# The first expert of mixture 1 split into two parts around the other seven, and a due table for two experts

## The reference

```python
x = attn_ref(x, weight).reshape(14336, 192)
# mixture 1
logits = x @ w_gate;  expert_idx = argmax(logits, 1);  gate_w = softmax(logits)[expert_idx]
for e in range(8):
    mask = expert_idx == e
    out[mask] = gate_w[mask, None] * (maximum(x[mask] @ w1[e], 0) @ w2[e])
# mixture 2, on the out of mixture 1
noisy = logits + log1p(exp(x @ w_noise)) * noise;  top2 = two largest;  top2_w = softmax over the two
for e in range(8):
    for k in range(2):
        mask = top2[:, k] == e
        out[mask] += top2_w[mask, k, None] * (maximum(x[mask] @ w1[e], 0) @ w2[e])
```

## Time and profile before

| | |
|---|---|
| median of 3 runs | 1960.8 us (1959.62 to 1962.15) |
| the profiled execution's own time | 1964.21 us |
| its span, first to last instruction | 1962.2 us |
| mean granted TensorE clock | 0.982 of full speed |
| TensorE matmuls busy | 1876.2 us, 96% of the span |
| VectorE / ScalarE / GpSimd busy | 1269.1 / 914.0 / 967.7 us |

### The profile page before, as it was taken

The page is one execution under the profiler, slowest core; times in us unless marked ns, Lnnn a source line. Parts: engine busy times, 40 slices in busy tenths (PEclk is TensorE's granted clock), DMA queues, the critical chain, the costliest instruction groups (busy, mean ns, idle before and its releaser), DMA issues.

```text
span 1962.2 us, 51451 instructions
## 1 busy us (share of the span) xinstructions
PE 1876.2 (96%) x14089; PEld 1821.5 (93%) x14090; DVE 1269.1 (65%) x4251; ACT 914.0 (47%) x2420; POOL 967.7 (49%) x1471
## 2 busy tenths in 40 slices
PE   8977599999999999799999999999999999999998
PEld 6657599999999999799999999999999999999998
DVE  5775488788887887655655655655655655655555
ACT  5543345555555455434444444444444444444444
POOL 4888554444444444444444444444444444444444
PEclk9979799999999999899999999999999999999999
DMA  7634243232332332322222222322322322322221
GB/s 274 230 113 128 74 127 120 89 115 79 117 118 84 116 100 92 103 74 62 81 78 62 85 74 62 104 63 63 102 62 64 96 64 66 97 62 86 78 63 48
DMA packets 113487, 185.23 MB, mean 94 GB/s; under 512 B 21675, under 2 KB 87971, under 8 KB 111287
## 3 DMA queue, kind: packets, MB, share of 16 engines
q1 hardware_dynamic: 73383, 104.53, 17.9%
q0 software_dynamic: 39936, 79.95, 12.6%
q10 hardware_dynamic: 144, 0.49, 0.1%
HBM read 111.34 MB, written 77.66 MB: 96 GB/s over the span
## 4 chain that ended last, share of the span: by engine, by line
PE 81%; issue 5%; DVE 5%; POOL 5%; ACT 1%; DMA 1%; DVEq 1%; ACTq 0%; POOLq 0%; SPq 0%
PE bank L1168 26%; PE bank L1169 12%; PE bank L1151 7%; PE bank L1153 7%; PE bank L1149 7%; PE bank L1152 7%; PE bank L1150 7%; POOL rows_of_mixture L1253 4%; PE bank L1138 2%; PE bank L1012 1%; DVE h_l L857 1%; PE bank L1139 1%; PE bank L1088 1%; POOL pause L1255 1%; DVE w1ml L666 1%
## 5 line engine op out<-in xcount | busy, mean ns | idle before, releaser
L1168 PE MATMUL bank<-w2hl,h_h 128*128 128x384 f32 (+1 forms) x2832 | 863.5, 370 | 14.4 <-DVE w2hl L672 6.7
L1169 PE MATMUL bank<-w2hl,h_l 128*128 128x192 f32 (+1 forms) x2832 | 721.1, 255 | 0.0
L857 DVE SCALAR_TENSOR_TENSOR h_l<-bank,h_h 128x512 fp32r<-128x512 f32 x708 | 477.5, 689 | 140.5 <-ACT h_h L565 101.2
L565 ACT ACTIVATE h_h<-bank 128x512 fp32r<-128x512 f32 x708 | 422.9, 598 | 301.2 <-PE bank L1153 261.6
L1168 PEld LDWEIGHTS bank<-w2hl,h_h 128*128 128x128 f32 x2832 | 534.0, 189 | 20.1 <-issue 12.6
L1169 PEld LDWEIGHTS bank<-w2hl,h_l 128*128 128x128 f32 x2832 | 543.1, 192 | 0.0
L1149 PE MATMUL bank<-x_h,w1mh 128*128 128x256 f32 x1416 | 401.7, 284 | 12.2 <-issue 9.5
L1280 POOL DMA_INDIRECT rows_of_mixture<-x_in,pos x248 | 245.7, 991 | 322.6 <-DVE h_l L857 110.0
L1151 PE MATMUL bank<-x_h,w1ml 128*128 128x256 f32 x1416 | 402.3, 284 | 0.5 <-issue 0.4
L1152 PE MATMUL bank<-x_h,w1lh 128*128 128x256 f32 x1416 | 400.1, 283 | 0.5 <-issue 0.5
L1153 PE MATMUL bank<-x_h,w1ll 128*128 128x256 f32 x1416 | 399.4, 282 | 0.2 <-issue 0.2
(11 more groups left out here) (199 smaller groups left out, 2017.0 us busy)
## 6 DMA issues: line engine op xcount, KB each, us to landing
rows<-rows_of_mixture SPq DMA_DIRECT2D x179, 208.0 KB
raw<-in_w_of_both SPq DMA_DIRECT2D x17, 1024.0 KB
raw<-in_w_of_both SPq DMA_DIRECT2D x17, 768.0 KB
out<-zeros SPq DMA_DIRECT2D x61, 192.0 KB
x_in<-in_x SPq DMA_DIRECT2D x15, 768.0 KB
raw<-in_moe_w_turned SPq DMA_DIRECT2D x8, 768.0 KB
rows_of_mixture<-pad_rows SPq DMA_DIRECT2D x21, 208.0 KB, 9.2
rows_of_mixture<-x_in,pos POOLq DMA_INDIRECT x248
```

Source lines behind the costliest of these rows:

```text
L565: nc.scalar.activation(h_h[:, 2 * p:2 * p + 2, :].rearrange("p c t -> p (c t)"), bank[1 + p][:], ACT.Relu).then_inc(hh_ready[m], 1)
L857: V.scalar_tensor_tensor(h_l[:, 2 * p:2 * p + 2, :].rearrange("p c t -> p (c t)"), bank[1 + p][:], 0.0, h_h[:, 2 * p:2 * p + 2, :].rearran ...
L1168: T.matmul(dst, h_h[:, c, tok], both, start=(c == 0), stop=False)
L1169: last = T.matmul(bank[5 + a][:, 0:width], h_l[:, c, tok], w2hl[:, c, 0:width], start=False, stop=(c == F // P - 1))
```

## The change

Mixture 1 is run in 9 parts instead of 8 experts (`PARTS = [E + 1, E]`). Part 0 is expert 0's first slots, at most four (`FIRST_SLOTS`) and at most all but one; parts 1 to 7 are the experts 1 to 7; part 8 is the rest of expert 0. With the counts above part 0 has 4 slots and part 8 has 2, so the number of slots stays 61. All engines loop over parts, and the running number of a set of weights becomes `PART0[m] + e`; expert 0's `w1` and `w2` are loaded and split a second time, for part 8. SP finds a part's first row in a new table `part_row`. `tables(0)` writes 9 entries instead of 8 and needs a fourth step in its running sum. The due table has a row for expert 0 and one for expert 1, so that SP waits for `slot_scattered` for the slots of both; the slots of part 2 and later still wait for all chunks.

```diff
+EARLY_EXPERTS = 2
+FIRST_SLOTS = 4
+PARTS = [E + 1, E]
+PART0 = [0, E + 1]
...
-                with sp_.Fori(0, E) as e:
+                def row_of(part, highest):
+
+                    if m == 1:
+                        return part * CAP
+                    return sp_.value_load(part_row[0:1, bass.ds(part, 1)], min_val=0, max_val=highest)
+
+                with sp_.Fori(0, PARTS[m]) as e:
...
-                                with sp_.If(e * WORD + j < EARLY - 1):
-                                    slot_scattered((j + 1) % EARLY)
+                                with sp_.If(e // EARLY_EXPERTS * WORD + j < EARLY - 1):
+                                    slot_scattered((e * E + j + 1) % (EARLY_EXPERTS * E))
...
-                            load_rows(e * CAP + j * SLOT + SLOT)
+                            load_rows(row_of(e, (E - 1) * CAP) + j * SLOT + SLOT)
                         with sp_.Else():
                             if m == 0:
-                                all_scattered()
+                                with sp_.If(e < 1):
+                                    slot_scattered(E)
+                                with sp_.Else():
+                                    all_scattered()
...
-                            load_rows((e + 1) * CAP)
-                        g = E * m + e
+                            load_rows(row_of(e + 1, E * CAP))
+                        g = PART0[m] + e
+                        following = (e + 1) % E + e // E * (E - 1) if m == 0 else (E + e + 1) % (2 * E)
                         with sp_.If(j < 1):
                             until((w1_ready, PAIRS * g + PAIRS))
-                            load_w1((g + 1) % (2 * E))
+                            load_w1(following)
...
-                    V.tensor_copy(first_count[:, k:k + 1], bank[2][0:1, RANKS:RANKS + 1])
+                    V.tensor_copy(first_count[:, :, k], bank[2][0:1, RANKS:RANKS + EARLY_EXPERTS])
...
+                parts = PARTS[m]
                 V.tensor_tensor(pad_at[m][:, 0:E], t_cnt[:], ecap[0:1, :], ALU.add)
-                V.memset(pad_at[m][:, E:E + 1], E * CAP).then_inc(pads_known[m], 1)
+                if m == 0:
+                    V.tensor_scalar(pad_at[m][:, E:E + 1], t_cnt[:, 0:1], float(SLOT), None, ALU.add)
+                V.memset(pad_at[m][:, parts:parts + 1], E * CAP).then_inc(pads_known[m], 1)
...
+                if m == 0:
+                    V.tensor_copy(part_row[:, 0:E], ecap[0:1, :])
+                    V.memset(part_row[:, E + 1:E + 2], E * CAP)
+                    V.tensor_scalar(slots[:, 1:E], t_shift[:, 1:E], 1.0, None, ALU.max)
+                    V.tensor_scalar(slots[:, E:E + 1], t_shift[:, 0:1], -float(FIRST_SLOTS), 1.0, ALU.add, ALU.max)
+                    link(V.tensor_scalar(t_first[:], t_shift[:, 0:1], -1.0, 1.0, ALU.add, ALU.max))
+                    link(V.tensor_scalar(slots[:, 0:1], t_first[:], float(FIRST_SLOTS), None, ALU.min))
+                    V.tensor_scalar(part_row[:, E:E + 1], slots[:, 0:1], float(SLOT), None, ALU.mult)
```

More of the change, by code:

```diff
@@ L61 @@
 WORD = 64
-C_TOTAL = E
+C_TOTAL = E + 1
 def empty_tiles(c):
@@ L154, in attention_and_two_mixtures @@
         c_pos = sb("c_pos", [TILE, XROW, CHUNK], i32)
-        slots_in = sb("slots_in", [1, E])
-        first_count = sb("first_count", [1, DUE_COLUMNS])
+        slots_in = sb("slots_in", [1, EARLY_EXPERTS, E])
+        first_count = sb("first_count", [1, EARLY_EXPERTS, DUE_COLUMNS])
         slot_full = sb("slot_full", [1, E])
-        slot_in = sb("slot_in", [1, DUE_COLUMNS, E])
+        slot_in = sb("slot_in", [1, EARLY_EXPERTS, DUE_COLUMNS, E])
         late = sb("late", [1, 1], i32)
-        due = sb("due", [1, E], i32)
+        due = sb("due", [1, EARLY_EXPERTS * E], i32)
         count2 = sb("count2", [P, SUBS, E], bf16)
-        one = [sb(f"one_{m + 1}", [1, E + 2], i32) for m in range(2)]
+        one = [sb(f"one_{m + 1}", [1, E + 3], i32) for m in range(2)]
         t_cnt = sb("t_cnt", [1, E])
         t_int, t_shift = sb("t_int", [1, E], i32), sb("t_shift", [1, E], i32)
-        t_word = sb("t_word", [1, E])
-        t_cum = sb("t_cum", [1, 3, 2 * E + 1])
-        pad_at = [sb(f"pad_at_{m + 1}", [1, E + 1], i32) for m in range(2)]
+        t_word = sb("t_word", [1, E + 1])
+        t_cum = sb("t_cum", [1, 3, 2 * E + 3])
+        t_first = sb("t_first", [1, 1])
+        part_row = sb("part_row", [1, E + 2], i32)
+        pad_at = [sb(f"pad_at_{m + 1}", [1, E + 2], i32) for m in range(2)]
         raw1 = sb("raw1", [P, 2, F])
@@ L356, in _ @@
                 else:
-                    sp_.wait_ge(late_ready, E)
+                    sp_.wait_ge(late_ready, PARTS[0])
                     missing = sp_.value_load(late[0:1, 0:1], min_val=0, max_val=1)
@@ L590, in body @@
                         if last:
-                            split_w1_h(E * m + e + 1, p)
+                            split_w1_h(PART0[m] + e + 1, p)
                         if p == 0 and m == 0:
@@ L618, in _ @@
                 total = total_of(act, m)
-                with act.Fori(0, E) as e:
+                with act.Fori(0, PARTS[m]) as e:
                     start, more = slots_of(act, m, e)
@@ L752, in early_slots @@
                 link = Steps(dve, dve_due)
-                shape = [1, DUE_COLUMNS, E]
+                shape = [1, EARLY_EXPERTS, DUE_COLUMNS, E]
                 link(V.tensor_scalar(slot_full[:], expert[0:1, :], float(SLOT), float(SLOT), ALU.mult, ALU.add))
-                link(V.tensor_tensor(slot_in[:], bc(first_count[:].unsqueeze(2), shape), bc(slot_full[:].unsqueeze(1), shape), ALU.is_ge))
-                link(V.reduce_sum(slots_in[:], slot_in[:].rearrange("p k j -> p j k"), AX.X))
-                V.tensor_scalar(due[:], slots_in[:], -1.0, float(CHUNKS), ALU.mult, ALU.add).then_inc(due_ready, 1)
+                link(V.tensor_tensor(slot_in[:], bc(first_count[:].unsqueeze(3), shape), bc(slot_full[:].unsqueeze(1).unsqueeze(1), shape), ALU.is_ge))
+                link(V.reduce_sum(slots_in[:], slot_in[:].rearrange("p s k j -> p s j k"), AX.X))
+                V.tensor_scalar(due[:], slots_in[:].rearrange("p s j -> p (s j)"), -1.0, float(CHUNKS), ALU.mult, ALU.add).then_inc(due_ready, 1)
             gate_to_low()
@@ L793, in tables @@
                 link(V.tensor_scalar(t_shift[:], t_int[:], SLOT.bit_length() - 1, None, ALU.arith_shift_right))
-                slots = t_cum[:, 0, E + 1:]
-                link(V.tensor_scalar(slots, t_shift[:], 1.0, None, ALU.max))
-                for i, step in enumerate((1, 2, 4)):
-                    a, b = t_cum[:, (0, 1, 2)[i], :], t_cum[:, (1, 2, 1)[i], :]
-                    link(V.tensor_tensor(b[:, E:], a[:, E:], a[:, E - step:2 * E + 1 - step], ALU.add))
-                before_e = t_cum[:, 1, E:]
@@ L800, in tables @@
-                link(V.scalar_tensor_tensor(t_word[:], before_e[:, 0:E], float(WORD), slots, ALU.mult, ALU.add))
-                V.tensor_scalar(one[m][:, 0:E], t_word[:], -1.0, None, ALU.add)
-                V.tensor_scalar(one[m][:, C_TOTAL + 1:C_TOTAL + 2], before_e[:, E:E + 1], -1.0, None, ALU.add)
-                V.tensor_copy(one[m][:, C_TOTAL:C_TOTAL + 1], before_e[:, E:E + 1]).then_inc(tables_ready[m], 1)
+                zero = E + 1
+                slots = t_cum[:, 0, zero + 1:zero + 1 + parts]
@@ new lines, in tables @@
+                if m == 0:
[6 more added lines that the diff above has]
+                    V.tensor_scalar(part_row[:, E:E + 1], slots[:, 0:1], float(SLOT), None, ALU.mult)
+                else:
+                    link(V.tensor_scalar(slots, t_shift[:], 1.0, None, ALU.max))
@@ new lines, in tables @@
+                end = zero + 1 + parts
+                turn = 0
+                for i, step in enumerate((1, 2, 4, 8)[:(parts - 1).bit_length()]):
+                    a, turn = t_cum[:, turn, :], (1, 2, 1, 2)[i]
+                    b = t_cum[:, turn, :]
+                    link(V.tensor_tensor(b[:, zero:end], a[:, zero:end], a[:, zero - step:end - step], ALU.add))
+                before_e = t_cum[:, turn, zero:end]
+                link(V.scalar_tensor_tensor(t_word[:, 0:parts], before_e[:, 0:parts], float(WORD), slots, ALU.mult, ALU.add))
@@ L804, in tables @@
+                V.tensor_scalar(one[m][:, 0:parts], t_word[:, 0:parts], -1.0, None, ALU.add)
+                V.tensor_scalar(one[m][:, C_TOTAL + 1:C_TOTAL + 2], before_e[:, parts:parts + 1], -1.0, None, ALU.add)
+                V.tensor_copy(one[m][:, C_TOTAL:C_TOTAL + 1], before_e[:, parts:parts + 1]).then_inc(tables_ready[m], 1)
                 return link
@@ L963, in _ @@
                 if m == 0:
-                    with dve.Fori(0, E) as e:
+                    with dve.Fori(0, PARTS[m]) as e:
                         start, more = slots_of(dve, m, e)
@@ L1192, in _ @@
                 total = total_of(pe, m)
-                with pe.Fori(0, E) as e:
+                with pe.Fori(0, PARTS[m]) as e:
```

20 lines of the change are left out of this document (10 added, 10 removed).

## The result

| | median of its runs | lowest to highest | span of the profiled execution |
|---|---|---|---|
| before | 1961.47 us (4) | 1959.62 to 1964.97 | 1962.2 us |
| after | 1929.32 us (4) | 1927.05 to 1931.65 | 1927.4 us |

The ratio is 0.9834, with an interval of 0.9816 to 0.9852: faster by 32.2 us, where 14.6 were forecast with a range of 7.3 to 22.8. The sign was right and the size was not. The rival "more than the stall comes back" had been priced at 1929.2 us. The forecast started from 1960.8 us, the median of three runs; a fourth of the kernel before took 1964.97 us, and the median of the four is 1961.47.

The account below looks back on a forecast made before the run. TensorE, 96% busy, was taken as the bound, with a stall at mixture 1's slot 4 rows paced by POOL's scatters. Sums of -17.5 and -11.7 us gave the middle, -14.6: 1946.2 us from 1960.8, range 1938 to 1953.5.

Parts of the forecast that it names:

- more than the stall comes back: Rival: slots 0 to 2 not slow without a profiler, so the stall was longer; -31.6 us, 1929.2 us, chance 0.10.
- What it removes: Mixture 1: no load waits for POOL any more, so TensorE's 23.3 us stall at slot 4's rows goes whole.
- The two paces: Mixture 1's slots after the stall's removal: slot 6's `y_b` 20.3 us sooner at full pace, 14.5 at slow pace.
- full pace: From slot 2's `y_b` at 192.8 us, plain slots take 10.0; slot 6 at 235.1, sum -17.5 us.
- the slow end: Late pace lasts until the last mark at 212.3 us; slot 6's `y_b` at 240.9, sum -11.7 us.
- the sum: Main case: gain from the removed stall less added costs, middle of both paces, -14.6 us; chance 0.68.
- the far rival: The rival "more than the stall comes back": -31.6 us, 1929.2 us, chance 0.10.
- Start of slot 0: Mixture 1's start: longer `tables(0)` 1.1 us and larger due table 0.2, together 1.3 us later.
- The change of weights: One more change in mixture 1: a first slot costs 2.0 us, a last slot 0.3, together 2.3 us.
- The `w2` load in the two-slot part: Part 8's last slot needs `w2` soon after its issue: barely hidden, 0 to 3 us, taken as 0.5.
- Slower: Rival: the pause at slot 3 ended the lateness; without it slots stay at 14.5 us, +19.8, 1980.6 us, chance 0.07.
- no effect: Rival: slot 4 still waits for all chunks, only added costs are paid; 1964.9 us, chance 0.05.

Follow-up runs that it names:

- e2: Kernel before with eight memsets on VectorE ahead of `tables(0)`, delaying mixture 1's slot 0: 1964.70 us, ratio 0.9997.
- e6: Kernel after with the nine parts but without the due table for expert 1, slot 4 waiting for all 15 chunks: 1964.47 us, ratio 1.0013.
- batch 3: Four runs on another chip, e9 to e12, with late signals; kernel before 1964.68 us over 8 runs, kernel after 1948.98 us.
- batch 2: Four runs, e5 to e8, without late signals; kernel before 1960.75 us over 13 runs, kernel after 1930.59 us.
- batch 4: Three runs on another chip, e13 to e15, with mild lateness: kernel after unedited 1938.07 us, zeros moved out of slots 0 to 7 1936.02, expert 1's weights later 1937.65.
- e11: Kernel after, unedited, third time, in batch 3: 1948.98 us, ratio 0.9916.
- e5: Kernel after, unedited, run once more in batch 2: 1930.59 us, ratio 0.9835.
- e10: Kernel after with eight memsets on VectorE ahead of `tables(0)`, in batch 3: 1955.40 us, ratio 0.9955.
- e7: Kernel after with `FIRST_SLOTS` 3 instead of 4, so parts 0 and 8 have three slots each: 1930.30 us, ratio 0.9842.
- e8: Kernel after with two memsets on VectorE ahead of `tables(0)`, a small delay of slot 0: 1931.99 us, ratio 0.9848.
- e9: Kernel before, unedited, profiled a third time, in batch 3: 1963.95 us.
- e12: Kernel after with only expert 1's first slot released early by the due table, in batch 3: 1957.33 us, ratio 0.9960.
- e13: Kernel after, unedited, fourth time, as the control in batch 4: 1938.07 us, ratio 0.9877.
- e15: Kernel after with expert 1's `w1` loaded in slot 1 and `w2` in slot 2, a slot later, in batch 4: 1937.65 us, ratio 0.9878.

## Why the prediction was wrong, point by point

**What it removes: right.** No load waits for the last mark, and TensorE's 23 us are gone. That no load waits for POOL at all was not quite so: slot 3's waits 5.8 us for an earlier mark. ScalarE then waits 1.5 us for the rows, and the slot in which this falls takes 10.37 instead of 10.0 us.

**The two paces: this step failed.** I took the pace of slots 0 to 2 from one profiled execution, and let it stand in both ends: even "full pace" began from slot 2's `y_b` at 191.51 and put it at 192.8. It came at 177.93, 14.9 us sooner. From there on the full pace was right to 0.1 us: 42.3 us were forecast up to slot 6's `y_b`, and 42.27 passed (177.93 to 220.20). The other 2.9 us of the miss are what the middle with the slow end took off the 17.5 of full pace. In the kernel before these slots lay ahead of a stall whose end the scatters fix, so no time bore on their pace; e2 shows this directly, with 9.4 us put ahead of the stall and nothing in the time. The pace is not the kernel's: the same program has slots of 10, 12 or 13.4 to 17.6 us by batch, and comes out at 1930.59, 1938.07 or 1948.98 us. The kernel before hardly shows it: 1960.75, 1962.97 and 1964.68 in the same batches, as its stall absorbs it (e6 shows such a stall with no late signal ahead of it, 34.7 us of TensorE's wait instead of 23.3).

Where the signals are late, the sum holds: in batch 3 the change gives 1964.68 - 1948.98 = 15.7 us, where I said 14.6, and slot 6's `y_b` comes at 237.74, inside the 235 to 241 named as the sign. Where they are not, the far rival holds: 30.2 us in batch 2 (1960.75 - 1930.59), 32.2 in the result, 31.6 priced. In batch 4, where they are mild, it gives 24.9 us (1962.97 - 1938.07), just beyond the range. That the result fell into a batch of the far kind was chance, and the rival would have missed in batch 3.

**The argument against that rival was no argument.** I wrote that a profiled execution only 3.4 us longer than the median shows that nothing else is slowed. But the kernel before hides the lateness, so such a difference can't speak on it. Nor does it tell which of its runs were late. The profiled 1964.21 fits the batches with late signals (1964.68, 1965.92) and the median of 1960.8 the one without (1960.75), but in the latter four of the 13 runs of the kernel before took 1964.88 to 1967.76 us, the other nine 1959.17 to 1962.27. No trace of the kernel before without late signals exists. What a late batch costs beyond the late slots themselves is small, by the spans 1.4 us in e11. From mixture 2's slot 3 on to the last, 112 slots, `y_b` goes in e11 and in e5 from the first row to the second:

```profile
846.74 0.73 ACT L576 ACTIVATE y_b<-bank,w_c 128x192 f32<-128x192 f32 x2 [3.60 <-PE bank L1201]
...
1938.94 0.73 ACT L576 ACTIVATE y_b<-bank,w_c 128x192 f32<-128x192 f32 x2
```
```profile
833.43 0.73 ACT L576 ACTIVATE y_b<-bank,w_c 128x192 f32<-128x192 f32 x2 [3.60 <-PE bank L1201]
...
1919.98 0.73 ACT L576 ACTIVATE y_b<-bank,w_c 128x192 f32<-128x192 f32 x2 [0.62 <-PE bank L1201]
```

1092.2 against 1086.6 us, 5.6 longer. Slot by slot both have 9.68 us nearly everywhere; e11 loses 0.5 to 0.9 us at each change of weights and next to nothing on balance elsewhere. e5 loses 4.3 us against e11 between the last slot of mixture 1 and this point, so the spans stay 17.6 + 5.6 - 4.3 = 18.9 apart, which is the 19.0 measured.

**Not the profiler alone.** The rival's mechanism, a slow pace in profiled executions only, is not what happened: profiled and other runs of one batch agree (e11: 1949.49 profiled, 1947.02 to 1949.84 the others), and five profiles have no late signals. Its arithmetic was right, its reason was not. That recording has no part in it is not shown, though: every run on record, profiled or not, comes with a span and a granted clock, and the traces of the two kinds differ in what was recorded (see the last section).

**The terms of what is added.** Start of slot 0: 1.3 forecast, 0.7 between the two profiles shown (144.77 against 144.08). The tables take 0.46 us more (2.60 against 2.14 between the first row's start and the last's), and the rest comes in ahead of them: the first row stands at 139.68 against 139.38. In batch 3 the start moved 1.6 us (145.05 against 143.42). The change of weights: first slots 12.1, last ones 10.1. The parts together: 3.7 by the medians of e6, 2.5 by its ratio, for 2.8. The `w2` load in the two-slot part: 0.3 us for 0.5. None of these is more than 1 us off.

**Slower, and no effect.** In no trace of the kernel after is a `y_b` late beyond slot 3, so the slower rival fell; its premise, that the pause had ended the lateness, fell with it, since in e11 it ends with no pause at all. What does go with its end is time: in all twelve traces with late signals every "remote" wait of over 1.5 us ends between 153 and 209 us, although slot 0 starts anywhere from 143.4 to 154.4. That is the stretch in which slots of mixture 1 run beside the last of POOL's 120 scatters (the 120th is issued at 209 to 212 us). In the kernel before the stall cuts it short. Slot 4 loads by the due table, as forecast.

**The rule on branches.** The Trainium skill, Runtime: NRT & Kernel Launch, section Instruction fetch mechanics, says that a taken branch to a target outside the fetched window costs a fetch. From it I had worked out that late signals would belong to the first passes through the slot's loop. The runs bear this out no better than the trace did: the same program has slots 0 to 2 late in e11 and none in e5, and with a start 9.5 us later (e10) slot 3 still has a "remote" wait of 2.2 us, at 208.02. Nor does e11 fetch more: the two instruction queues on the profile's page read 7 and 18 packets in both. Whether a fetch takes longer there can't be seen.

**What stays open** is what makes TensorE's signals late in one batch and not in another. It is not POOL's scatters alone (the same 12.4 us of them in both windows above), not the order of the program, not the chip alone, since batches 1 and 2 shared one, and in batch 2 a start 2.0 us later did not bring it on. Taking away the transfers of zeros or shifting those of weights did not end it where it was mild. The recording of the runs stands as an untested rival.

## What to carry to other kernels

When a change removes a wait whose end something else fixes, what comes back is not the wait's length but the distance to where the work would have been without it, and the pace ahead of the wait is then a term that the time of the kernel before has never tested. Price it at the engine's own pace as well as at the one recorded, with real weight on both, and ask whether the pace is marked "remote" or otherwise unexplained. Put a delay ahead of the wait if you can: if the time does not move, it says nothing on the pace there. Take a few us between a profiled execution and the median as a question and not as comfort, and compare versions only within one batch on one chip: here the kernel after spread over 18 us between batches and over 3 to 5 within one. Two others spread wider in batch 2, the kernel before over 8.6 us and e7 over 14.6, so one batch need not be all of one kind.

## What the runs showed of the hardware

TensorE's completions can reach ScalarE and VectorE up to some 5 us behind its recorded matmuls, between about 150 and 210 us of this program, in one batch of runs and not in the next, at a granted clock that reads 1.00 where it was first seen. Whether the matmuls or only their signals are late is not shown, as a matmul's end is modelled; the starts run on 0.12 us apart. All profiles of a batch agree in it, but one of e7's runs, 9 us above its other three, may have been of the other kind; it has no trace.

There is a sign of it in the profile's page. The landing of the `pad_rows` transfer, in the section on DMA issues (KB each, median us to landing), reads in e5 and in e11:

```profile
rows_of_mixture<-pad_rows SPq DMA_DIRECT2D x22, 208.0 KB, 2.1
```
```profile
rows_of_mixture<-pad_rows SPq DMA_DIRECT2D x22, 208.0 KB, 9.1
```

It is 2.1 us in all five profiles without late signals (after, e5 to e8) and 9.1 or 9.2 in the twelve others, the profile of the kernel before among them; batch 4, where the lateness is mild, reads 9.1 too. But the transfer is not slower. The 22 issues stand on two lines, three on L325 near 15 us and 19 on L341 later. In the kernel after the first row below is L325's, the second L341's:

```profile
DMA to landing us min/median/max: 8.4/9.1/9.4
```
```profile
DMA to landing us min/median/max: 2.0/2.1/3.8
```

e11 has the same row for L325 and none for L341: there the 9.1 is the median of the three early ones alone, and the landings of the other 19 can't be told. SP's own wait for this transfer, 1.8 us in the kernel after and 1.7 in e11, says the same. What differs is what was recorded. Counted in the traces themselves, those without late signals hold 25514 to 25661 updates of semaphores, the twelve others 16635 to 17272, with as many instructions (51832 in e5 and in e11). From 160 to 200 us, where the signals are late, e5 has 786 of them and e11 213, about a quarter; from 300 to 1900 us, where nothing is late, it is 19799 and 13563, about two thirds. So lost records and late signals go together by the kind of run, and the loss is greatest where the lateness is. Which of the two makes the other, or what makes both, is not shown.
